# Whole-row key loads, reciprocals turned by TensorE, sums added by GpSimd, and new order tables in an attention and feed-forward kernel

## The reference

```
q_pool = q.reshape(B, H, S // 2, 2, D).mean(axis=3)
scores = matmul(q_pool, k.T) / sqrt(D);  scores -= max(scores)
attn = exp(scores);  attn /= sum(attn) + 1e-9
x = matmul(attn, v)                        # -> 2304 tokens x 512
h = x @ w_in;  g = where(h >= 1, h, where(h <= -1, 0, (h + 1)**2 / 4));  y = g @ w_out
out = max(y @ w1, y @ w2, y @ w3) @ w_out2
```

## Time and profile before

| | us |
|---|---|
| median of 3 runs | 1243.48 (1241.06 to 1243.55) |
| the profiled execution | 1244.4 |
| its span, first to last instruction | 1242.7 |
| PE busy | 1223.2 (98%) |
| DVE busy | 732.5 (59%) |
| ACT busy | 618.2 (50%) |
| POOL busy | 274.7 (22%) |
| granted TensorE clock, mean | 0.997 |

### The profile page before, as it was taken

How to read it: one execution, slowest core, us unless ns; L and a number is a source line. 1 busy time by engine, 2 the same in 40 slices (tenths; PEclk the granted TensorE clock), 3 DMA queues, 4 the chain that set the end, 5 groups by cost and what they waited for, 6 DMA issues and landing times.

```text
span 1242.7 us, 19281 instructions
## 1 busy us (share of the span) xinstructions
PE 1223.2 (98%) x7061; PEld 1074.9 (87%) x7061; DVE 732.5 (59%) x1508; ACT 618.2 (50%) x1433; POOL 274.7 (22%) x240
## 2 busy tenths in 40 slices
PE   7999999999999999999999999999999999999998
PEld 6999999999999999878888888888898878787887
DVE  5999999999999999853443443443452132212222
ACT  5898899889988998832222222222331111112011
POOL 3133333333333333379000000000192000000000
PEclk8999999999999999999999999999999999999999
DMA  3565656666666664434100000000041010101010
GB/s 95 96 114 114 116 115 116 116 115 116 116 115 115 113 116 79 78 98 143 30 1 1 1 1 1 1 1 1 2 136 33 1 34 1 35 1 35 1 35 17
DMA packets 124604, 76.17 MB, mean 61 GB/s; under 512 B 62560, under 2 KB 111712, under 8 KB 124512
## 3 DMA queue, kind: packets, MB, share of 16 engines
q1 hardware_dynamic: 124512, 74.94, 29.8%
HBM read 47.71 MB, written 4.79 MB: 42 GB/s over the span
## 4 chain that ended last, share of the span: by engine, by line
PE 94%; DVE 2%; ACT 2%; issue 0%; SPq 0%; DMA 0%; POOL 0%; DVEq 0%; ACTq 0%
PE hid L936 34%; PE acc L962 16%; PE values L519 12%; PE trans L437 11%; PE scores L502 7%; PE scores L503 6%; PE acc L994 5%; PE trans L457 1%; PE trans L447 1%; DVE neg_max_parts L649 1%; DVE pT_lo L663 1%; ACT probs L568 1%; ACT qT L1027 0%; ACT pT_hi L559 0%; DVE qT L1033 0%
## 5 line engine op out<-in xcount | busy, mean ns | idle before, releaser
L936 PE MATMUL hid<-qT,w_slots 128*128 128x512 f32 (+1 forms) x1680 | 367.8, 372 | 0.0
L936 PEld LDWEIGHTS hid<-qT,w_slots 128*128 128x128 f32 x1680 | 293.6, 188 | 61.2
L649 DVE TENSOR_REDUCE neg_max_parts<-scores 128x1 f32<-128x384 f32 x432 | 227.1, 550 | 8.9 <-PE scores L503 4.3
L663 DVE TENSOR_TENSOR pT_lo<-trans,pT_hi 128x384 fp32r<-128x384 f32 x432 | 225.7, 546 | 5.0 <-ACT pT_hi L559 4.4
L559 ACT ACTIVATE pT_hi<-trans 128x384 fp32r<-128x384 f32 x432 | 205.8, 494 | 42.0 <-PE trans L437 38.8
L568 ACT ACTIVATE probs<-scores,neg_max 128x768 f32<-128x768 f32 (+1 forms) x288 | 212.5, 742 | 6.5 <-DVE neg_max L656 5.6
L437 PE MATMUL trans<-ident,probs 128*128 128x128 f32 x1296 | 201.0, 275 | 4.9 <-DVE pT_lo L663 2.8
L502 PE MATMUL scores<-kT,qT 128*128 128x384 f32 x480 | 182.4, 380 | 2.0 <-ACT probs L568 1.5
L437 PEld LDWEIGHTS trans<-ident,probs 128*128 128x128 f32 x1296 | 155.9, 140 | 20.5 <-DVE pT_lo L663 8.9
L503 PE MATMUL scores<-kT,qT 128*128 128x384 f32 x480 | 162.6, 339 | 0.0
L1059 ACT ACTIVATE excess<-rise,halves 128x512 f32<-128x512 f32 (+1 forms) x80 | 54.5, 681 | 185.9 <-DVE rise L1129 185.9
(11 more groups left out here) (77 smaller groups left out, 1494.2 us busy)
## 6 DMA issues: line engine op xcount, KB each, us to landing
kT<-k_split SPq DMA_DIRECT2D x60, 288.0 KB, 5.4
k_raw<-in_k SPq DMA_DIRECT2D x32, 288.0 KB, 6.1
v_raw<-in_v SPq DMA_DIRECT2D x32, 288.0 KB
q_raw<-in_q SPq DMA_DIRECT2D x32, 256.0 KB, 3.2
k_split<-value_all SPq DMA_DIRECT2D x64, 72.0 KB, 2.9
out<-X SPq DMA_DIRECT2D x18, 256.0 KB, 2.9
q_raw<-in_moe_w_out SPq DMA_DIRECT2D x14, 256.0 KB, 3.1
k_raw<-in_moe_w SPq DMA_DIRECT2D x12, 256.0 KB, 3.2
```

The costliest lines, as they stand in the source:

```text
L649: dve.tensor_reduce(neg_max_parts[:, par, n:n + 1], scores[:, score_banks(s)[n], 0:SB], AX_X, ALU.max, negate=True).then_inc(parts_done, 1)
L663: dve.tensor_tensor(*tile_places(pT[1], src, s % TILES, g), hi.bitcast(F32), ALU.subtract).then_inc(p_lo_done, 1)
L936: last = pe.matmul(out_bank, weight(slot, part, half, k), x[:, k, cols], start=(k == 0 and part == 0 and x is x_hi), stop=(k == KC - 1 and ...
```

## The change

Five things are changed, all but the tables at the places that the diff shows.

1. `load_k` is one DMA for both heads; the destination keeps each partition's rows as they lie in DRAM, 2304 bytes a piece, where two DMAs wrote pieces of 256 bytes.
2. A key transpose so takes two neighbouring key blocks of one head. Odd blocks come to lie ahead of even ones (`KEY_BLOCKS`), and `place_k` needs 6 DMAs with the same bytes (3 for each part) in place of 4.
3. The sum of the exponentials' two halves and the 1e-9 go from DVE to a new GpSimd step, `safe_total`, of two 128x9 instructions (L395, L397). It stands after `head_values` 0 on GpSimd's list and, for the last pair, after `add_values` 1. DVE's `R` is the reciprocal alone (L751) and waits for it.
4. The reciprocals are transposed by PE (new step `R`, one transpose), copied from PSUM to `recips_turned` (9 rows of 128) by ACT (new step `R`) and sent to DRAM in pieces of 512 bytes. The last pair's transpose is PE's last step before the feed-forward products.
5. The three tables are new. `K0` to `K2` come later (tiles 1 to 3, before 0 to 2), and DVE's `R` comes after the maxima of the next tile.

```
 PE_ORDER = """
-S1.2 S1.0 K0
-T0.0 W2:10-14 S2.0 T0.1 W2:14-16 T0.2 S2.1 W2:16-18 S2.2 K1 S3.0 W3:0-9
+S1.2 S1.0
+T0.0 T0.1 W2:10-13 S2.0 W2:13-16 T0.2 W2:16-18 S2.1 S2.2
+T1.0 T1.1 W3:0-3 S3.0 W3:3-8 R W3:8-9 S3.1 S3.2 K0 T1.2
...
         def load_k(pair):
-            for h in range(2):
-                src = k_heads[bass.ds(head(pair) + h, 1)].rearrange("h p (t d) -> p (h t) d", d=D)
-                sp.dma_start(k_raw[:, :, h, :], src).then_inc(k_loaded, 16)
+            src = k_pairs[bass.ds(head(pair) // 2, 1)].rearrange("c p h n -> p (c h) n")
+            sp.dma_start(k_raw.rearrange("p h t d -> p h (t d)"), src).then_inc(k_loaded, 16)
...
-            for h in range(2):
-                for a in range(2):
-                    copy_parts(sp, kT[rows_of(a), pair % 2, h, :], k_parts[rows_of(h), a, :], k_placed)
+            places = kT[:, pair % 2].rearrange("p h s -> p (h s)")
+            for a in range(2):
+                copy_parts(sp, places[rows_of(a), ODD:ODD + S], k_parts[rows_of(0), a, :], k_placed)
+                copy_parts(sp, places[rows_of(a), 0:ODD], k_parts[rows_of(1), a, 0:ODD], k_placed)
+                copy_parts(sp, places[rows_of(a), ODD + S:2 * S], k_parts[rows_of(1), a, ODD:S], k_placed)
...
-            sp.wait_ge(recip_done, pair + 1)
-            sp.dma_start(recip_rows[pair % 2].rearrange("(t p) -> p t", p=P), recips[:],
-                         allow_slow_non_contiguous=True).then_inc(recip_sent, 16)
+            sp.wait_ge(recip_kept, pair + 1)
+            sp.dma_start(recip_rows[pair % 2].rearrange("(t p) -> t p", p=P), recips_turned[:]).then_inc(recip_sent, 16)
...
+        def safe_total(pair):
+
+            pool.wait_ge(exp_done, (pair + 1) * (2 * TILES))
+            if pair > 0:
+                pool.wait_ge(recip_done, pair)
+            par = pair % 2
+            pool.tensor_tensor(safe_sums[:], sums[:, par, 0], sums[:, par, 1], ALU.add).then_inc(sums_added, 1)
+            pool.wait_ge(sums_added, pair + 1)
+            pool.tensor_scalar(safe_sums[:], safe_sums[:], 1.0, 1e-9, ALU.mult, ALU.add).then_inc(safe_done, 1)
...
             if i > 0:
-                add_values(i - 1, 2, (v_ready, 2 * i + 1))
+                safe_total(i - 1)
+                add_values(i - 1, 2, (safe_done, i))
...
             add_values(i, 1)
+        safe_total(PAIRS - 1)
         split_weights(2)
...
+        def recip_transposes(pair):
+
+            group = ("R", pair, 0)
+            wait_bank(group)
+            pe.wait_ge(recip_done, pair + 1)
+            pe.transpose(trans[0:TILES, BANK[group], 0:P], recips[:], ident[:]).then_inc(recip_trans_done, 1)
...
+        recip_transposes(PAIRS - 1)
...
+        def keep_recips(pair):
+
+            act.wait_ge(recip_trans_done, pair + 1)
+            if pair > 0:
+                act.wait_ge(recip_sent, 16 * pair)
+            act.activation(recips_turned[:], trans[0:TILES, BANK["R", pair, 0], 0:P], ACT.Copy).then_inc(recip_kept, 1)
...
         def reciprocals(pair):
 
-            dve.wait_ge(exp_done, (pair + 1) * (2 * TILES))
+            dve.wait_ge(safe_done, pair + 1)
             if pair > 0:
-                dve.wait_ge(recip_sent, 16 * pair)
-            par = pair % 2
-            dve.scalar_tensor_tensor(out=safe_sums[:], in0=sums[:, par, 0], scalar=1e-9, in1=sums[:, par, 1],
-                                     op0=ALU.add, op1=ALU.add).then_inc(safe_done, 1)
-            dve.wait_ge(safe_done, pair + 1)
+                dve.wait_ge(recip_trans_done, pair)
             dve.reciprocal(recips[:], safe_sums[:]).then_inc(recip_done, 1)
```

93 lines of the change are left out of this document (53 added, 40 removed).

## The result

The changed kernel takes 1260.4 us (median of 4 runs, 1257.6 to 1268.2) beside 1243.5 us for the kernel before on the same chip (1241.1 to 1243.9). The ratio is 1.015, with an interval of 1.012 to 1.017. It is slower by 16.9 us, where the forecast was 25 slower, in a range of 1244 to 1293.

A forecast was written before the change was run, and what follows sets the result against it. TensorE was taken to carry the span (94%), with VectorE and ScalarE nearly full. The terms 20.8 + 1.0 - 0.3 + 4.0 - 0.6 = +25 us on the median of 1243.5 gave 1269 us, range 1244 to 1293.

The forecast's parts named there:

- rival A: The forecast itself: VectorE waits for GpSimd's sums in each pair, 1256 to 1282 us; chance 0.69.
- B: The chain shortens by 3.7 us or more, so the sums come in time: 1240 us; chance 0.13.
- C: Nothing is saved on the chain, with six placements and the same bytes: period 35.4, 1295 us; chance 0.10.
- D: Only the wait at the end stays, the middle neither gains nor loses: 1247 us; chance 0.08.
- When VectorE wants the sums: In each pair, the time VectorE's reciprocal needs the sums: 21.3 us after the placing of the keys.
- GpSimd's chain at the old DMA times: In each pair, GpSimd's sums without any DMA saving would come 25.5 us after the placing.
- The two small steps: GpSimd's two new sum steps with their handovers: 0.5 us, between 0.2 and 1.6.
- What the change saves on the chain: DMA time saved from the placing to GpSimd's sums by cheaper keys and no four-byte send: 2.0 us.
- The period: Pairs 2 to 14: the loop takes 33.4 us against 31.8, 13 x 1.6 = 20.8 us more.
- Pair 1 and pair 15: First and last chains: +1.0 us for half a full wait, -0.3 for the removed addition.
- The end: Where the feed-forward layers begin, TensorE waits for VectorE behind the late last reciprocal: +4.0 us.
- The start: GpSimd's first queries, which stand behind the key load, come earlier: 0 to 1 us, taken as -0.6.

The follow-up runs named there:

- e1: The changed kernel with GpSimd's two sum steps ahead of the values' split instead of behind it: 1241.4 us, ratio 0.996.
- e3: The kernel before with only the sums moved to GpSimd behind the values' split, old tables, key loads and four-byte send: 1305.8 us, ratio 1.047.
- e4: The changed kernel with one idle GpSimd step between the two sum steps in each pair but the last: 1280.0 us, ratio 1.027.
- e11: The changed kernel with the two sum steps ahead of the values' split, run once more with more rounds: 1241.7 us, ratio 0.998.
- e8: The kernel before with late sums on GpSimd and keys loaded as whole rows, old tables and four-byte send: 1297.5 us, ratio 1.041.
- e9: The changed kernel with the old tables, the reciprocals' transposition and copy put later than in e7: 1304.2 us, ratio 1.048.
- e2: The changed kernel with the sum back on VectorE as one two-input step right ahead of the reciprocal: 1248.3 us, ratio 1.001.
- e12: The changed kernel with the sum on VectorE as a reduction and a second step of one input each: 1251.5 us, ratio 1.003.
- e5: The kernel before with only the whole-row key load, its six placements, block order and key waits: 1244.2 us, ratio 0.998.
- e7: The changed kernel with the old tables, the reciprocals' transposition and copy put behind the second key group: 1328.0 us, ratio 1.066.

## Why the prediction was right, and where it wasn't

- **The mechanism** (rival A) was right, and e1, e3 and e4 show it. B (the chain is short enough), C (nothing is saved) and D (only the end) are out: VectorE waits 15 times, and the middle costs 13.1 us where the span has grown by 13.2.
- **When VectorE wants the sums**: place + 21.3 forecast. Where nothing is waited for (e1, e11) it is 21.75. Off by 0.45; the sum took the reciprocal's position from counted steps, and a tile end was an estimate.
- **GpSimd's chain at the old DMA times**: 25.5 forecast, 25.3 in e3. Right.
- **The two small steps**: 0.5 forecast, 0.50 measured. Right, with nothing of that kind in the trace of before.
- **What the change saves on the chain**: 2.0 forecast, 25.28 - 23.10 = 2.2 measured. The number was right by luck and its reason wrong. The keys gave 0.2 and not 0.9 (e8 against e3), the send 0.2 and not up to 1 (e9 against e8), and 1.7 came from the tables (changed against e9), which stand at nothing in the sum. I had said that the new order was hidden by the same wait; but K2, Q2 and the placing lie on the ring, and there no step has cover. The working also didn't ask what SyncE's query load waits for. Nor did the lower price of the keys' bytes show anywhere: quarter 3 came no earlier for them.
- **The period**: 33.4 forecast, 32.75 measured. 23.1 + 9.75 in place of 23.5 + 9.9, and 0.1 less because the last of the 14 is short. Over the middle it is 13.1 us in place of 20.8: this is the term that was mis-sized most, by 7.7. The forecast took 13 periods of 1.6 more; the same 13 measured 13.8, and the last one, the pair 15 of the next point, took 0.7 back.
- **Pair 1 and pair 15**: +1.0 - 0.3 forecast, together +0.9 measured. This is only what is left of the 12.0 us by which the feed-forward layers start later, after the middle (14 periods), the start and the end: the first reciprocal comes 1.85 later in spite of the earlier start, and the last two reciprocals are 2.2 closer together. e1, which has no waits in the pairs, shows nearly the same (1.5 later and 2.0 closer), so it goes with the reciprocal's new place in the pair. Near, but no row confirms the two terms by themselves.
- **The end**: +4.0 forecast, -0.8 measured. Wrong in sign. I read the 4.82 us of the two pieces of the first tile's rest as their own length. They are 1.22 each in the changed kernel, where GpSimd is idle. In the kernel before they alternated with GpSimd: the first piece was held until GpSimd's weight split ended, the row below, at 528.42 + 2.36 = 530.78; it then held GpSimd's adding of quarter 1 (1.78 us, elsewhere 0.80), and that the second piece. e2 and e12 show this exclusion by itself. Since the last sums stand behind GpSimd's steps, VectorE now comes when GpSimd is through, and the forecast wait of TensorE is gone; what is left of the term, -0.8, is a length between two rows neither of which waits for the other. GpSimd's timeline in the kernel before:

```profile
528.42 2.36 POOL L903 TENSOR_TENSOR w_slots<-q_raw,w_slots 128x1024 fp32r<-128x1024 f32 x1
```

- **The start**: -0.6 forecast, -1.2 measured: GpSimd's first query step starts at 6.91 where it was 8.10, and e5 has 7.10 with the keys alone.
- **What no term covers**: 1.2 us more in the feed-forward layers, and 3.7 by which the medians differ more than the two spans. The account is 24.9 forecast, - 7.7 in the middle, - 4.8 at the end, - 0.6 at the start, + 0.2 for pairs 1 and 15, + 1.2 + 3.7 = 16.9 measured. So part of the nearness of 1269 to 1260.4 is owed to these last two and is luck: the 3.7 are the spread of the executions, and for the 1.2 no run looks.
- **What would show it**: reciprocal waits of 2 us some 14 times (1.25 us, 15 times), a key load issue under 1 us (0.59), quarter 3 at place + 11.8 (11.1 to 12.3, though not by the keys) came, the waits shorter than forecast; the wait of TensorE at the start of the feed-forward layers didn't.

## What to carry to other kernels

Before a small step moves to an idle-looking engine, read what that engine's idle time waits for and where in its queue the step will stand: with the same two instructions of 0.2 us behind a 2 us split the kernel is 17 us slower than before, with them ahead of it 2 to 6 us faster. Once somebody waits for a chain, every member of it counts, table entries and the waits of the DMA queue too, and steps that were rightly hidden before have no cover left. A late ring can cost twice, as in e3, e4 and e7 to e9, where TensorE's clock fell after some of its stops. And before the duration of a VectorE or GpSimd step is used as a price, look at what the other one did at that time; the same step beside an idle neighbour gives its own length.

## What the runs showed of the hardware

- VectorE's two-input addition of 128x9 elements takes 0.16 to 0.17 us, and up to 1.40 while GpSimd runs its steps; it ends with GpSimd's. A `tensor_scalar` of that size behaves alike (0.17 to 1.24), a reduction (0.165 to 0.177) and a reciprocal (0.20 to 0.22, also where it lies inside GpSimd's split, as 19 times in e1 and e11) do not.
- It goes both ways: GpSimd's adding of 64x288 elements took 1.78 us in place of 0.80 while VectorE's two-input rest was running.
- GpSimd's smallest steps, 128x9 elements, take 0.20 to 0.21 us, and 0.09 pass from one to a dependent one (320.15 + 0.20 to 320.44).
- A load in runs of 2,304 bytes in place of 256 cut the packets from 124,604 to 93,980 (e5; the send in rows of 512 bytes took the rest, to 75,581) and the issue from 2.70 to 0.59 us, and was worth 0.2 us on the chain and 1.2 us at the start.
- After TensorE had stood for 2.70 us (e4) its granted clock was 0.50 for about 3 us and the stretch from reciprocal to placing took 11.1 us in place of 9.7; after another of 2.21 us, and one of 3.25, it stayed full.
